# A fused attention and expert kernel: the routing between the two stages redone

## What is computed

```python
logits = np.einsum('bsd,de->bse', x, w_gate)
local_gate = 1.0 / (1.0 + np.exp(-np.einsum('bsd,de->bse', x, w_local).squeeze(-1)))
for b in range(B):
    prev_e = -1
    for s in range(S):
        fresh_e = int(np.argmax(logits[b, s]))
        if s == 0 or local_gate[b, s] < 0.5:
            e = fresh_e
        else:
            e = prev_e if prev_e >= 0 else fresh_e
        prev_e = e
        ls = logits[b, s] - logits[b, s].max()
        p = np.exp(ls)
        p /= p.sum() + 1e-09
        h = np.maximum(x[b, s] @ w1[e], 0.0)
        out[b, s] = p[e] * (h @ w2[e])
```

## Time and profile before

| | us |
|---|---|
| median of 3 runs | 564.8 (561.66 to 565.51) |
| profiled execution | 565.11 |
| its span, first to last instruction | 562.3 |
| mean granted TensorE clock | 0.93 |

### The profile page before, as it was taken

How to read it: one execution, slowest core, us unless ns; L and a number is a source line. 1 busy time by engine, 2 the same in 40 slices (tenths; PEclk the granted TensorE clock), 3 DMA queues, 4 the chain that set the end, 5 groups by cost and what they waited for, 6 DMA issues and landing times.

```text
span 562.3 us, 11139 instructions
## 1 busy us (share of the span) xinstructions
PE 491.4 (87%) x4348; PEld 303.2 (54%) x4348; DVE 291.3 (52%) x415; ACT 290.6 (52%) x267; POOL 336.2 (60%) x175
## 2 busy tenths in 40 slices
PE   4769999999999999975831669999999999999993
PEld 2436777767676767754620345455555555555541
DVE  4654666666666666511856341654454544545441
ACT  3066978787878787983250500094865958000000
POOL 1246788787878787897301986068969759500011
PEclk9998999999999999997555787999999999999998
DMA  6694555555336332000920137255382562200000
GB/s 156 158 259 134 139 149 147 148 150 150 74 76 186 76 71 50 5 1 1 346 68 6 51 95 198 91 217 209 146 317 94 221 225 93 84 14 20 5 1 0
DMA packets 55842, 65.12 MB, mean 116 GB/s; under 512 B 31395, under 2 KB 39983, under 8 KB 55794
## 3 DMA queue, kind: packets, MB, share of 16 engines
q1 hardware_dynamic: 52754, 56.29, 32.9%
q0 software_dynamic: 3040, 8.13, 4.7%
HBM read 47.99 MB, written 8.13 MB: 100 GB/s over the span
## 4 chain that ended last, share of the span: by engine, by line
PE 55%; POOL 15%; ACT 10%; DVE 8%; issue 5%; DMA 3%; another core or an unknown queue 2%; SPq 1%; ACTq 0%; DVEq 0%; POOLq 0%
PE pO L1035 17%; PE pA L1035 16%; POOL room L402 8%; POOL W L291 7%; ACT room L569 5%; ACT room L575 3%; PE pB L1053 3%; PE pA L466 2%; PE pA L467 2%; PE pB L483 2%; PE pB L484 2%; DMA room<-room 2%; DVE room L650 1%; PE pP L1025 1%
## 5 line engine op out<-in xcount | busy, mean ns | idle before, releaser
L402 POOL TENSOR_TENSOR room<-room 128x1536 f16<-128x1536 f32 x48 | 148.9, 3102 | 43.7 <-ACT room L575 43.5
L291 POOL TENSOR_TENSOR W<-room,W 128x1024 f16<-128x1024 f32 x64 | 135.0, 2133 | 41.9 <-ACT W L283 41.7
L277 ACT ACTIVATE room<-W 128x1024 f32<-128x1024 f32 x64 | 64.7, 1047 | 101.2 <-DMA W<-in_moe_w 69.6
L650 DVE TENSOR_REDUCE room<-pA 128x2 f32<-128x1536 f32 x46 | 80.8, 1757 | 55.6 <-PE pA L467 55.6
L1035 PE MATMUL pO<-W,room 128*128 x456 | 104.0, 385 | 3.0 <-DVE room L1115 3.0
L1035 PE MATMUL pA<-W,room 128*128 x456 | 103.4, 383 | 2.7 <-DVE room L1103 1.7
L569 ACT ACTIVATE room<-pB 128x1536 f32<-128x1536 f32 x48 | 69.3, 1444 | 36.5 <-PE pB L484 31.9
L1035 PEld LDWEIGHTS pO<-W,room 128*128 128x128 f16 x456 | 45.3, 99 | 54.9 <-issue 6.7
L1035 PEld LDWEIGHTS pA<-W,room 128*128 128x128 f16 x456 | 45.0, 99 | 54.3 <-issue 6.0
L575 ACT ACTIVATE room<-room 128x1536 f16<-128x1536 f32 x48 | 71.2, 1484 | 1.5
L521 PE MATMUL pO<-W,room 128*128 128x64 f16 x576 | 63.7, 194 | 5.5 <-POOL room L402 5.4
(11 more groups left out here) (185 smaller groups left out, 647.3 us busy)
## 6 DMA issues: line engine op xcount, KB each, us to landing
W<-in_moe_w SPq DMA_DIRECT2D x32, 1024.0 KB, 9.3
room<-room SPq DMA_DIRECT2D x96, 96.0 KB, 2.9
room<-in_q SPq DMA_DIRECT2D x16, 192.0 KB, 3.3
room<-in_k SPq DMA_DIRECT2D x16, 192.0 KB, 3.2
W<-in_v SPq DMA_DIRECT2D x4, 768.0 KB, 5.5
x_rows<-XN SPq DMA_DIRECT2D x12, 256.0 KB, 3.4
room<-room SPq DMA_DIRECT2D x32, 18.0 KB
room<-room SPq DMA_DIRECT2D x32, 1.5 KB
```

The source lines that it names most:

```text
L291: pool.tensor_tensor(parts(r)[:, 1, cols], FULL[:, place(r), cols], parts(r)[:, 0, cols], ALU.subtract).then_inc(s_ready, 1)
L402: pool.tensor_tensor(PTL[:, n % NP, :, :], E32[:, n % 2, :, :], PTH[:, n % NP, :, :], ALU.subtract).then_inc(s_lo, 1)
L650: dve.reduce_max(RM[:, g % 2, 2 * p:2 * p + 2], scores_in(n)[:, :].rearrange("p (i s) -> p i s", i=2), AX.X).then_inc(s_rmax, 1)
```

## The change

- **Logits.** The first six chunks of the logits, those of sequence 0, are made inside the attention loop: in steps 44 to 49 TensorE turns chunk i, VectorE makes both parts, and one step later (45 to 50) TensorE makes its products. They are placed after `scores` and before `values(n - 2)`. They use pA, free by then, and the room of T1 and T2. The other six (sequence 1) follow the last norm, with three buffers instead of two; there ScalarE makes the high parts (`high_rows_act`) ahead of its work on weight round 7, and VectorE the low parts. WGH and WGL are made in step 9.
- **Fill.** Each partition scans its own 6 tokens per sequence (`LS`: 24 elements, product of factors and local result); TensorE turns the ends to two rows of 128, VectorE scans these (`CR`), TensorE turns the carries back, and a product and a sum give the experts `EB`. SP's six transfers are gone. Masks MK are made by GpSimd.
- **Ranks.** OH is float16; one triangle product and twelve products with ones, of falling width, in float16 into one accumulation, give ranks and totals over the chunks at once. Some of VectorE's instructions go.
- **Slots.** Token numbers count from 1, and 0 marks an empty slot, so the table product has 19 columns instead of 38; the gathers wait only for FROM.
- **Gates.** They are made right after xc(0), ahead of relu(0). The gate is scaled and split in three float16 parts GP; the product is float16 with 57 columns, with the selection ROWH that exists already, and the three parts are summed afterwards. ROWOH is gone.

```diff
+                i = n - TAIL
+                if 0 < i <= NC // 2:
+                    logits(pe, i - 1)
+                if 0 <= i < NC // 2:
+                    if i == 0:
+                        pe.wait_ge(s_wgp, 2)
+                        pe.wait_ge(s_rmax, NS)
+                        pe.wait_ge(s_x, NH // B)
+                    turn_rows(pe, i)
                 if pair(n - LAG):
                     values(n - LAG)
...
+        def turn_rows(pe, i):
+            c, buf, before = logits_of(i)
+            wait(pe, s_gc, before)
+            for d in range(DC):
+                last = pe.transpose(pG[buf][:, d * P:(d + 1) * P], XN[:, c, d * P:(d + 1) * P], idf[:, :])
+            last.then_inc(s_gt, 1)
+
+        def logits(pe, i):
+            c, buf, _ = logits_of(i)
+            pe.wait_ge(s_gc, i + 1)
+            for d in range(DC):
+                for m, (a, r) in enumerate(((0, WGL), (1, WGH), (0, WGH))):
+                    last = pe.matmul(pL[:, c * (E + 1):(c + 1) * (E + 1)], XTC[:, buf, a, d * P:(d + 1) * P], r[:, d, :],
+                                     start=d == m == 0, stop=d == DC - 1 and m == 2)
+            last.then_inc(s_gl, 1)
...
             act.wait_ge(s_x, NH)
+            for i in range(NC // 2, NC):
+                high_rows_act(act, i)
             scale_weights(act, EARLY, 0)
...
+            for i in range(NC // 2, NC):
+                turn_rows(pe, i)
+                if i > NC // 2 + 1:
+                    logits(pe, i - 2)
+            logits(pe, NC - 2)
+            logits(pe, NC - 1)
+
+            pe.wait_ge(s_loc, 1)
+            for a in range(2):
+                last = pe.transpose(pS[0:B, a * P:(a + 1) * P], LS[:, a, :, J - 1], idf[:, :])
+            last.then_inc(s_end, 1)
+            pe.wait_ge(s_carry, 1)
+            pe.transpose(pR[:, 0:B], CR[0:B, 0:P], idf[0:B, 0:B]).then_inc(s_back, 1)
...
+            pe.matmul(pR[:, 128:128 + NC * E], upper16[:, :], ohf, start=True, stop=False, skip_group_check=True)
+            for k in range(1, NC + 1):
+                last = pe.matmul(pR[:, 128 + k * E:128 + (NC + 1) * E], ones16[:, :], ohf[:, 0:(NC + 1 - k) * E],
+                                 start=False, stop=k == NC, skip_group_check=True)
+            last.then_inc(s_rk, 1)
...
-            dve.wait_ge(s_rowd, 16 * 2 * B)
-
-            dve.tensor_tensor_scan(ROWS[:, 2, :], ROWS[:, 0, :], ROWS[:, 1, :], 0.0, ALU.mult, ALU.add).then_inc(s_scan, 1)
-            dve.wait_ge(s_eb, 16 * B)
+            dve.tensor_tensor_scan(flat(LS), flat(SA), flat(SV), 0.0, ALU.mult, ALU.add).then_inc(s_loc, 1)
+            dve.wait_ge(s_end, 1)
+            ch.link(dve.tensor_copy(AR[0:B, :], pS[0:B, P:2 * P]))
+            dve.tensor_tensor_scan(CR[0:B, 1:P + 1], AR[0:B, :], pS[0:B, 0:P], 0.0, ALU.mult, ALU.add).then_inc(s_carry, 1)
+            dve.wait_ge(s_back, 1)
...
-            dve.tensor_copy(FROM[:, :], pP[:, 0:NT])
-            ch.link(dve.tensor_scalar(FAR[:, :], pP[:, NT:2 * NT], -float(4 * T), float(4 * T), ALU.mult, ALU.add))
-            dve.tensor_tensor(TO[:, :], FAR[:, :], pP[:, 0:NT], ALU.add).then_inc(s_slot, 1)
+            dve.tensor_scalar(FROM[:, :], pP[:, 0:NT], -1.0, 0.0, ALU.add, ALU.max).then_inc(s_slot, 1)
...
             pe.wait_ge(s_by, 2)
             for c in range(NC):
-                last = pe.matmul(pT[0][:, 0:NT], ROWOH[:, c, :], BG[:, c, :], start=c == 0, stop=c == NC - 1)
+                last = pe.matmul(pL[:, 0:3 * NT], ROWH[:, c, :], BG[:, c, :, :].rearrange("p a t -> p (a t)"),
+                                 start=c == 0, stop=c == NC - 1)
             last.then_inc(s_map, 1)
```

More of the change, by code:

```diff
@@ L247, in prep_in, with logits_of, high_rows, high_rows_act @@
             return pO if g < AHEAD and half == 1 else pP
+        pG = [pA[:, 0:512], pA[:, 512:1024], pB[:, 0:512]]
+        pL = pA[:, 1024:1536]
+        def logits_of(i):
+            half = NC // 2
+            if i < half:
+                return i * B, i % 2, i - 1
+            return (i - half) * B + 1, i % 3, i - 1 if i < half + 2 else 0 if i == half + 2 else i - 2
+        def turn_rows(pe, i):
[12 more added lines that the diff above has]
+            last.then_inc(s_gl, 1)
+        def high_rows(dve, i):
+            _, buf, before = logits_of(i)
+            dve.wait_ge(s_gt, i + 1)
+            wait(dve, s_gl, before)
+            dve.tensor_scalar(XTC[:, buf, 0, :], pG[buf][:, 0:DM], XS, None, ALU.mult).then_inc(s_gh, 1)
+        def high_rows_act(act, i):
+            _, buf, before = logits_of(i)
+            act.wait_ge(s_gt, i + 1)
+            wait(act, s_gl, before)
+            act.activation(XTC[:, buf, 0, :], pG[buf][:, 0:DM], ACT.Copy, scale=XS).then_inc(s_gh, 1)
+        def low_rows(dve, i):
+            _, buf, _ = logits_of(i)
+            dve.wait_ge(s_gh, i + 1)
+            dve.scalar_tensor_tensor(XTC[:, buf, 1, :], pG[buf][:, 0:DM], XS, XTC[:, buf, 0, :],
+                                     ALU.mult, ALU.subtract).then_inc(s_gc, 1)
+        TAIL = NS - LEAD + 1
         def head(g):
@@ L704, in _ @@
                     bits(h + 3, 1)
-        pG = [pA, pB]
-        pT = [pA[:, 1024:1536], pB[:, 1024:1536]]
-        pL = pO
+                if p == 0 and h == 3:
+                    dve.wait_ge(s_wg, 16 * 2 * DC)
+                    dve.tensor_scalar(WGH[:, :, :], wg[:, :, :], WS, None, ALU.mult).then_inc(s_wgp, 1)
+                    dve.wait_ge(s_wgp, 1)
+                    dve.scalar_tensor_tensor(WGL[:, :, :], wg[:, :, :], WS, WGH[:, :, :],
+                                             ALU.mult, ALU.subtract).then_inc(s_wgp, 1)
+                i = n - TAIL
+                if 0 <= i < NC // 2:
+                    if i == 0:
+                        dve.wait_ge(s_asm[(NH - 1) % NQ], 96 * ((NH - 1) // NQ + 1))
+                        dve.wait_ge(s_asm[(NH - 2) % NQ], 96 * ((NH - 2) // NQ + 1))
+                    high_rows(dve, i)
+                    low_rows(dve, i)
+        pS, pR = pO, pB[:, 512:1024]
         low_at = Layout(full_at.at)
@@ L1121, in _ @@
             xc(0)
-            relu(0)
-            xc(1)
-            hc(0)
-            relu(1)
             ch = Chain(dve, s_gw)
-            dve.tensor_tensor(ROWOH, *rows, ALU.is_equal)
             dve.wait_ge(s_ex, 1)
```

164 lines of the change are left out of this document (77 added, 87 removed).

## The result

The changed kernel takes 545.61 us (median of 4 runs, 543.93 to 546.06) against 563.93 us; the ratio is 0.9673, with a 95% interval of 0.9631 to 0.9715. The sign was right, and the range of 530 to 546 us held by 0.4 us only; the gain in the profiled spans was 19.2 us where the sum said 29.8.

The account below looks back on a forecast made before the run. Bound: GpSimd in the last attention steps, then serial work from last head to first gather, then the delay before down(1). Gains 8.4 + 6.1 + 2.1 + 13.2 = 29.8 us off 565.1 give 535.3 us; range 530 to 546.

Parts of the forecast that it names:

- Part 1, logits: Logits: six chunks move into attention steps, ScalarE makes the second half's high parts; gain 8.4 us, lower bound 6.4.
- the possibility that the prediction kept for its lower end: Second half of the logits: TensorE at full clock, chunks costing about half, up to 4 us less.
- the 24.4 us: Whole sum, instead of 29.8, if ScalarE's logits passes took 2.1 us each by the skill's rule; the prediction rejected it.
- rival C: Attention tail not free: TensorE's queue waits behind unconverted chunks; three of five costing 2.9 us give 544; chance 0.08.
- Part 2, fill: Fill over rows between logits and ranks: no transfers, 4.85 us instead of 10.97; gain 6.1 us.
- cover of 5.0 us for round 7: GpSimd's part of weight round 7: free at 285.3, before the new first gather at 290.3.
- Part 3: Ranks and slots before the first gather: shorter products and VectorE chain, fewer waits; gain 2.1 us (1.6 to 2.3).
- Part 4, gates: First gather to down(1): float16 gate product, VectorE's gates hidden under up(0); gain 13.2 us, down to 8.5 or 10.8.
- The end: Tiles from down(1) on: run back to back, 11.67 us each, so bringing down(1) forward brings the end forward.
- Rivals A: Whole kernel: the forecast itself, the four gains arrive, 531 to 540 us; chance 0.72.
- Rival B: First tiles don't tighten: late take-up or low clock at down(0) costs 4 to 5 us, 539 to 545; chance 0.15.
- the unexplained 351.26: Kernel before: down(0)'s result taken up only at 351.26, its last product started by 347.0; 0.3 us left for it.

Follow-up runs that it names:

- round 7 late: Changed kernel with GpSimd's two subtractions of weight round 7 moved from the start of the fill to behind the first three gathers: 554.5 us, ratio 0.9837.
- gates late: Changed kernel with VectorE's gates put back behind relu(1), the float16 product staying where it is: 549.2 us, ratio 0.9723.

## Why the prediction was right in sign and 10 us off

- **Part 1, logits: mechanism right, 2.0 us more than the sum.** Of these 0.4 us are an earlier end of the last norm, which varies by more than that. The clock did come up in the second half (0.64 against 0.50), the possibility that the prediction kept for its lower end. ScalarE's pass of 512 columns took 0.60 (0.58 forecast, from the two rows of PSUM passes); not 2.1. (The figure of three times in the Trainium skill, ScalarE: Activation LUTs, Rules for kernel authors, is given there for bf16 in VectorE's fastest mode, so it did not bear on this float32 pass from PSUM; the 24.4 us worked out from it lay nearer by accident.) Nothing of the tail came late by rival C's 8.7 us, since the last norm ended at 266.58 (266.99 before) and in no variant later than 267.73: rival C is out.
- **Part 2, fill: 2.15 us short.** The instruction costs were right (with GpSimd elsewhere the fill is 4.69 us against 4.85, and the product with the mask 0.26 against 0.28). What failed is the cover of 5.0 us for round 7: the prediction asked only whether GpSimd would be free for the gathers, not whose instructions its two subtractions lie beside.
- **Part 3: right,** 2.3 against 2.1.
- **Part 4, gates: 4.2 us instead of 13.2.** The failed step is "about 3.1 us, under up(0), which takes over 5.4. Not on the path". The price was taken from rows in which GpSimd made no subtractions; beside its eight subtractions the block cost 15.7 us, and relu(0) came 8.4 us after the end of up(0). Without that wait and without a stall the same stretch gained 14.0. The move from behind relu(1) to ahead of relu(0) put it there. The earlier trace rows held the warning: before, GpSimd's subtractions end at 327.40 and the old gates start at 329.89. The product itself was as forecast (0.51 us in 0.45 to 0.8), as was the clock at down(0) (5.34 us).
- **The end: 1.5 us,** the last down at a lower clock (0.78), after a wait of 2.66 us for VectorE, where it ran at the full one before after the same wait. Nothing in the change touches it, and both durations occur among the variants (5.35 us in five of them, 6.8 to 7.0 in six, one profile each). The sum had the end at nothing; its cause stays open.
- **Rivals A and B.** The forecast's own 531 to 540 failed. Rival B, 539 to 545, came within 0.6 us, but by luck: it named the unexplained 351.26 or a low clock at down(0), and the changed kernel has neither a late take-up nor a slow down(0). The wait itself was real and came back, longer, in six variants.

Without both collisions and without the row of gathers the forecast comes out in sum: 562.9 for the kernel before with its gathers spread, 532.8 for the changed one with gathers spread, gates in PSUM and round 7 late, a difference of 30.1 us against 29.8. The agreement is partly of errors that cancel: part 1 gave 2 us more, the last down took 1.5 more, and moving round 7 showed 1.0 us of its 2.6.

## What to carry to other kernels

The price of a small instruction of VectorE from a stretch without GpSimd's passes doesn't hold beside them: before moving VectorE work, look at what GpSimd does at the new place, and put one operand into PSUM where a move can't avoid it. Ask of each engine moved or delayed what it will lie beside, not only whether it ends in time. When a removed wait gives nothing back, compare what the engine waits for next; here it was a row of sixteen gathers, and breaking the row into eights was worth 16 us once the gates no longer waited. In the changed kernel itself, where the row stalled nothing, breaking it up was worth nothing that can be told from none (545.6 to 544.9).

## What the runs showed of the hardware

- Beside GpSimd's 128x1024 subtractions of 2.08 us a 128x12 instruction of VectorE between SBUF operands takes 2.06 us, against 0.20 alone. One input in PSUM, or the result of a form with one input, is enough to escape it (0.20); sums over columns (0.28), reciprocals (0.26) and the setting of constants (0.12) escape too.
- It seems to work the other way round as well, though no run varied this alone: in the kernel before, one gather's issue (330.06) took 2.40 us beside VectorE's selection of 1536 elements with two SBUF inputs (329.89), where its neighbours took 0.95; with the gates late, one (316.60) took 1.64 us beside a product of 684 elements that started at 316.55.
- Sixteen gathers of 128 rows, issued 1.25 us apart, held up TensorE's issue and its semaphores by 7 to 13 us in six kernels, until shortly before their last data landed, by under 1 us in one and not at all in another; eight gathers did not, nor eight gathers and four scatters in a row beside weight loads at 338 GB/s.
